# Slot weights of a fused attention and two-MoE kernel: ten parts loaded early, a ring in the order of use, filler products on TensorE

## The reference

```python
x = attention(q, k, v)          # 4 x 8 heads x 576 positions x 64, window of 128 keys, ALiBi bias
x = x.reshape(2304, 512)
# first MoE: 32 slots, 4 per expert ("slot" weights moe_w1, moe_w2)
logits = x @ phi                                  # 2304 x 32
d = softmax over tokens(logits);  slot_input = d.T @ x          # 32 x 512
for e in range(8):                                # 4 slots each
    slot_out[e] = relu(slot_input[e] @ w1[e]) @ w2[e]           # 512 x 1024, 1024 x 512
y = softmax over slots(logits) @ slot_out         # 2304 x 512
# second MoE: all tokens through all 8 experts ("big" weights moe2_w1, moe2_w2)
P = 8 Sinkhorn rounds of exp(y @ w_gate)
out = sum over e of P[:, e] * (relu(y @ w1[e]) @ w2[e])
```

## Time and profile before

| what | value |
|---|---|
| median of 3 runs | 1057.57 us (1056.58 to 1058.82) |
| the profiled execution: its time | 1057.44 us |
| its span, first to last instruction | 1055.5 us |
| outside the span | 1.94 us |
| mean granted TensorE clock | 0.969 |
| PE busy | 1005.1 us, 95% of the span |
| DMA, mean | 83 GB/s |

### The profile page before, as it was taken

One profiled execution on the slowest core, in us unless ns is written; L12 is line 12 of the kernel. 1 busy time (PEld: TensorE's weight loads), 2 busy tenths in 40 slices (PEclk: granted clock), 3 DMA queues, 4 the chain that ended last, 5 costly groups with the idle time before them and its releaser, 6 DMA issues.

```text
span 1055.5 us, 25401 instructions
## 1 busy us (share of the span) xinstructions
PE 1005.1 (95%) x8599; PEld 924.3 (88%) x8599; DVE 748.2 (71%) x1994; ACT 583.7 (55%) x1368; POOL 615.1 (58%) x522
## 2 busy tenths in 40 slices
PE   7999979579999999999999999999999999999998
PEld 5888843029999999999999999999999999999998
DVE  7767741426898867876867778778768777877675
ACT  6777710224466746555655566466546564656552
POOL 6445410004487648684966596568747873877443
PEclk9999988658999999999999999999999999999999
DMA  5773267950200220022002200210040012000111
GB/s 184 262 277 112 71 273 265 408 209 2 81 1 2 81 81 2 2 82 81 2 3 83 81 2 2 99 63 1 14 148 5 2 72 91 2 2 20 61 41 61
DMA packets 36904, 87.81 MB, mean 83 GB/s; under 512 B 2976, under 2 KB 2976, under 8 KB 36768
## 3 DMA queue, kind: packets, MB, share of 16 engines
q1 hardware_dynamic: 36768, 86.07, 22.4%
HBM read 81.35 MB, written 4.72 MB: 82 GB/s over the span
## 4 chain that ended last, share of the span: by engine, by line
PE 41%; POOL 27%; issue 22%; DMA 4%; DVE 4%; ACT 1%; POOLq 1%; ACTq 0%; DVEq 0%
POOL s_split L499 19%; PE bank L775 8%; PE bank L777 7%; PE bank L779 7%; POOL t_split L504 4%; PE bank L568 3%; PE bank L578 3%; PE bank L597 3%; DMA late_raw<-slot_w_in 3%; PE bank L725 2%; PE bank L678 2%; PE bank L615 1%; POOL raw L533 1%; POOL raw L535 1%; POOL raw L537 1%
## 5 line engine op out<-in xcount | busy, mean ns | idle before, releaser
L499 POOL TENSOR_TENSOR s_split<-s_sum,s_split 128x512 fp32r<-128x512 f32 x288 | 372.5, 1309 | 342.2 <-ACT s_split L887 337.0
L1241 DVE SCALAR_TENSOR_TENSOR acc<-bank,gate_now,acc 128x256 f32<-128x256 f32 x441 | 228.6, 519 | 146.8 <-PE bank L779 145.8
L887 ACT ACTIVATE s_split<-s_sum 128x512 fp32r<-128x512 f32 x288 | 181.8, 632 | 247.6 <-PE bank L779 137.8
L775 PE MATMUL bank<-t_split,s_split 128*128 128x256 f32 x1008 | 284.2, 282 | 1.3 <-DVE acc L1235 1.1
L777 PE MATMUL bank<-t_split,s_split 128*128 128x256 f32 x1008 | 282.6, 280 | 0.0
L779 PE MATMUL bank<-t_split,s_split 128*128 128x256 f32 x1008 | 282.6, 280 | 0.0
L775 PEld LDWEIGHTS bank<-t_split,s_split 128*128 128x128 f32 x1008 | 189.4, 188 | 5.1 <-issue 3.4
L779 PEld LDWEIGHTS bank<-t_split,s_split 128*128 128x128 f32 x1008 | 192.6, 191 | 0.0
L777 PEld LDWEIGHTS bank<-t_split,s_split 128*128 128x128 f32 x1008 | 189.4, 188 | 0.0
L775 PE MATMUL bank<-t_split,a 128*128 128x256 f32 x576 | 164.1, 285 | 5.8 <-DVE acc L1235 2.5
L777 PE MATMUL bank<-t_split,a 128*128 128x256 f32 x576 | 162.6, 282 | 0.0
(11 more groups left out here) (167 smaller groups left out, 1952.5 us busy)
## 6 DMA issues: line engine op xcount, KB each, us to landing
raw<-big_w_in SPq DMA_DIRECT2D x15, 2048.0 KB, 8.6
early_raw<-slot_w_in SPq DMA_DIRECT2D x12, 1024.0 KB, 10.5
late_raw<-slot_w_in SPq DMA_DIRECT2D x10, 1024.0 KB, 13.5
slot_raw<-slot_w_in SPq DMA_DIRECT2D x7, 1024.0 KB, 5.2
q_ring<-q_tiles SPq DMA_DIRECT2D x18, 256.0 KB, 4.6
k_ring<-k_tiles SPq DMA_DIRECT2D x18, 256.0 KB, 4.9
v_ring<-v_rows SPq DMA_DIRECT2D x18, 256.0 KB, 2.7
out_rows<-acc SPq DMA_DIRECT2D x18, 256.0 KB, 2.0
```

What stands on the lines that cost most here:

```text
L499: pool.tensor_tensor(s_split[:, i, 1, :, :], s_sum[:, i, :, :], s_split[:, i, 0, :, :].bitcast(F32), ALU.subtract)\
L775: pe.matmul(to, left[:, 0, f, :], t_place(parity, k, 0)[:, f, :], start=(f == 0 and k in FRESH), stop=False, skip_group_check=k not in FRESH)
L887: act.activation(s_split[:, i, 0, :, :], s_sum[:, i, :, :], ACT.Copy).then_inc(s_hi_ready, 1)
L1241: done = dve.scalar_tensor_tensor(out=to, in0=got, scalar=gate, in1=to, op0=ALU.mult, op1=ALU.add)
```

## The change

The masked bias copy is gone: for the two mixed tiles DVE sets the masked quarter of each score tile and reads the plain bias in two pieces. Its room and some more takes three buffers `mid_raw`, so that ten parts are loaded during attention. Three parts (`early_raw`) follow at the end of attention and four (`late_raw`) behind `x_used`: 17 buffers. From part 17 on the buffers are used again in the order in which PE frees them, from part 0's on, without those of parts 13 and 14, which hold `w2_first`, now issued behind part 23. ACT's first weight split waits until 24 parts are used. PE makes six filler products (128 columns of weights, 512 moving columns, result never read) before each of the last eight parts, four after the last part, four before it waits for the slot outputs and twelve after the first hidden blocks. On DVE the remainders of the first pair of tiles come ahead of its sums.

```diff
     RAW_RING = 7
-    EARLY_RAW = 4
-    EXTRA_RAW = 1
+    MID_RAW = 3
+    EARLY_RAW = 3
     LATE_RAW = 4
+    PREFETCHED = RAW_RING + MID_RAW
...
-        return n if n < BUFFERS else RAW_RING + (n - BUFFERS) % AGAIN
+        return n if n < BUFFERS else n - BUFFERS if n - BUFFERS < FIRST_LATE else n - BUFFERS + SKIPPED
...
-    W2_FIRST_AFTER = BUFFERS + 2
+    W2_FIRST_AFTER = BUFFERS + RAW_RING - 1
+    FILL_FROM = BUFFERS + RAW_RING
+    SKIPPED = 2
...
                 if n >= BUFFERS:
-                    sp.wait_ge(part_used, n - AGAIN + 1)
+                    sp.wait_ge(part_used, buffer_of(n) + 1)
...
                 if n == W2_FIRST_AFTER:
-                    sp.wait_ge(comb_t_ready, (TILES + 3) // 4)
+                    sp.wait_ge(part_used, FIRST_LATE + SKIPPED)
                     sp.dma_start(w2_first[:, :, :], rows_first(moe_w2[0])).then_inc(w2_loaded, 16)
...
-            pool.wait_ge(bias_ready, HEADS)
-            pool.tensor_copy(bias_mixed[:, :, :], bias[:, :, :]).then_inc(mixed_ready, 1)
-            pool.wait_ge(mixed_ready, 1)
-            pool.memset(bias_mixed[P // 2:P, :, 0:P + P // 2], MASKED / SCALE).then_inc(mixed_ready, 1)
...
+            def fill(count):
+
+                for _ in range(count):
+                    pe.matmul(bank[7][:, :], c_stack[:, 0:P], c_stack[:, 0:512], start=True, stop=True)
...
             for n in range(PARTS // 2, PARTS):
+                if n == FILL_FROM:
+                    pe.wait_ge(comb_lo_ready, (TILES + 3) // 4)
+                if n >= FILL_FROM:
+                    fill(6)
                 part_products(bank[5], hid_wide, lambda g: n % 2 * (FT // 2) + g, n, n == PARTS // 2, n == PARTS - 1)
+            fill(4)
             pe.wait_ge(rows_copied, 2)
...
+            fill(4)
             pe.wait_ge(so_split, 1)
...
             for s in range(2):
                 hidden(0, 0, 0, s, 0, 0)
+            fill_late(12)
...
             act.wait_ge(w2_loaded, 16)
+            act.wait_ge(part_used, BUFFERS + RAW_RING)
...
+                    if t % PERIOD == MIXED:
+
+                        dve.memset(scores[P // 2:P, r, n, 0:P + P // 2], -MASKED)
+                        parts = [(slice(0, P // 2), cols), (slice(P // 2, P), slice(P + P // 2, 2 * P))]
...
             for s in range(2):
+                a11_low(0, s)
+            for s in range(2):
+                a2_low(0, 0, s)
+            for s in range(2):
                 sums_first(0, 0, s, 0)
                 sums_second(0, 0, s, 0)
```

More of the change, by code:

```diff
@@ L710, in g_products, with fill_late @@
                 last.then_inc(g_ready, 1)
+            def fill_late(count):
+                for _ in range(count):
+                    pe.matmul(bank[0][:, :], c_stack[:, 0:P], c_stack[:, 0:512], start=True, stop=True)
             def hidden(e, p, parity, s, n, before):
@@ L983, in bias_pair @@
                     dve.wait_ge(probs_t_ready, GROUP_PAIRS * (g - SCORE_RING + 1))
-                biases = bias_mixed if t % PERIOD == MIXED else bias
-                if g == 2 * MIXED and p == 0:
-                    dve.wait_ge(mixed_ready, 2)
                 for n in range(2 * p, 2 * p + 2):
@@ L991, in bias_pair @@
                         dve.memset(scores[:, r, n, 0:P // 2], -MASKED)
-                    dve.tensor_tensor_reduce(
-                        out=scores[:, r, n, cols], in0=bank[n][:, cols], in1=biases[:, GROUP_HEADS * (g % 2) + n, cols],
-                        scale=-SCALE, scalar=3e38, op0=ALU.add, op1=ALU.min, accum_out=neg_max[:, r, n:n + 1]).then_inc(scores_read, 1)
+                    parts = [(slice(0, P), cols)]
+                    if t % PERIOD == MIXED:
+                        dve.memset(scores[P // 2:P, r, n, 0:P + P // 2], -MASKED)
+                        parts = [(slice(0, P // 2), cols), (slice(P // 2, P), slice(P + P // 2, 2 * P))]
+                    for rows, cs in parts:
+                        done = dve.tensor_tensor_reduce(
+                            out=scores[rows, r, n, cs], in0=bank[n][rows, cs], in1=bias[rows, GROUP_HEADS * (g % 2) + n, cs],
+                            scale=-SCALE, scalar=3e38, op0=ALU.add, op1=ALU.min, accum_out=neg_max[rows, r, n:n + 1])
+                    done.then_inc(scores_read, 1)
             def invert_sums(g):
@@ L1151, in sums_first @@
                                          op0=ALU.max, op1=ALU.add).then_inc(s_sum_ready, 1)
-                rounded, rest = [a2[:, slot, lo, blocks_f, :, :].rearrange("p f t c -> p (f t c)") for lo in range(2)]
-                dve.scalar_tensor_tensor(out=rest, in0=bank[4 + 2 * s][:, :], scalar=0.0, in1=rounded.bitcast(F32),
-                                         op0=ALU.max, op1=ALU.subtract)\
-                   .then_inc(a2_lo_ready, 1)
+                if before:
+                    a2_low(n, slot, s)
                 dve.wait_ge(s_sum_ready, 8 * n + 4 * s + 1)
@@ L1170, in sums_second @@
                                          op0=ALU.max, op1=ALU.add).then_inc(s_sum_ready, 1)
-                dve.scalar_tensor_tensor(out=a11[:, 1, blocks_f, :], in0=first_half(s)[:, :, 0, :], scalar=0.0,
-                                         in1=a11[:, 0, blocks_f, :].bitcast(F32), op0=ALU.max, op1=ALU.subtract)\
-                   .then_inc(a11_lo_ready, 1)
+                if before:
+                    a11_low(n, s)
             kept = gates[:, 0:TILES, 0:GATES]
```

73 lines of the change are left out of this document (40 added, 33 removed).

## The result

The changed kernel takes 1047.0 us (median of 4, 1046.21 to 1048.19), the kernel before 1058.11 us beside it (median of 4, 1056.58 to 1058.82). The ratio is 0.990, its 95% interval 0.9886 to 0.9915: faster by some 11 us. The forecast was -17.2 us; 1047.0 is the upper end of the range. The profiled execution took 1046.21 us, with a span of 1044.2 (before 1055.5) and a mean clock of 0.989 (before 0.969).

A forecast was written before the change was run, and what follows sets the result against it. PE, busy 95% of the span, bounds the kernel, and the load stream bounds W2. -12.5 - 2.45 - 1.45 - 0.8 = -17.2 us on 1057.44 gives 1040.3 us; 8 in 10 range 1036.5 to 1047.0.

The forecast's parts named there:

- The ring and the stream: W2's loads: first reload 9.0 us sooner and 17 units instead of 18, last part at full clock, -12.5 us.
- a step above 2.56: Sign of being wrong, last eight parts of W2: a step of fillers and part longer than the DMA's 2.56 us.
- The split of w2_first: ACT and DVE during W2: split ends at 204 us, 6 us ahead of the last part, costing nothing.
- From the last part to g: Fillers, fold and g after W2 run at full clock, 4.6 us instead of 7.05: -2.45 us.
- From g to A12: From G, the end of g, to A12's end: late fillers raise the clock, -1.45 us; new order brings nothing.
- The rival of a cold tail: After W2: stream gains as forecast, but the tail stays at low clock and fillers there cost 3.9 us: 1048, 14%.
- The start: Start of attention: without POOL's memset of the masked copy, DVE's first step is shorter, -0.8 us.
- Mixed tiles: Attention's mixed tiles: DVE's additional 0.3 us a score, 1.2 a quad, stays below its 1.46 us wait, costing nothing.
- The rival named this mechanism: Attention's mixed tiles cost: DVE loses 3 to 5 us over four quads, total 1043 to 1045, 10%.
- if PE pauses in the mixed tiles: Sign of being wrong in attention, where mixed tiles were claimed to cost nothing.
- The second MoE can't be changed: Nearly all of the span, PE busy 95%: the edits can't change it, so no gain or loss there.

The follow-up runs named there:

- experiment 4: The changed kernel with each reload of the ring waiting for seven parts more than it needs: 1057.93 us, ratio 0.9999 to the kernel before.
- experiment 5: The changed kernel with seven parts loaded in attention instead of ten, still 17 buffers: 1052.25 us, ratio 0.9948 to the kernel before.
- experiment 6: The changed kernel without any filler product, between the parts, in the tail or ahead of A11: 1051.0 us, ratio 0.9938 to the kernel before.
- experiment 3: The changed kernel with DVE's order of the first pair's remainders, and its code in the expert loop, put back as before: 1047.54 us.
- experiment 11: The changed kernel with the masked bias copy kept, nine parts loaded in attention, and POOL writing the masked quarter first: 1042.41 us.
- experiments 1 and 2: First: changed kernel with masked copy kept, nine parts loaded in attention, 1042.21 us. Second: kernel before with two-piece mixed tiles, no copy, 1062.13 us.
- Experiments 8 to 10: In order: changed kernel without twelve late fillers, 1056.42 us; with them cut to 8 columns, 1050.7; with copy kept plus 48 DVE memsets, 1044.35.

## Why the prediction was right and where it failed

The direction was right, and so was the largest mechanism. By its own steps:

**The ring and the stream: right.** -12.5 us forecast, -11.9 measured from the start of the slot parts. The late reload, put back by itself, costs 10.3 us (experiment 4), and taking the three parts out of attention 3.4 (experiment 5). The two come to more than 11.9, since each also brought a cold first step of fillers, 1.8 and 1.6 us. The seventeenth buffer was in both and had no run of its own. Of the 0.6 us missing, 0.4 are there before any filler counts: part 24 was forecast 32.0 us behind the slot parts (161.65 + 4.47 + 10 x 2.56 - 159.69) and starts 32.4 behind. The other 0.2 are the step of PE, 7 x 0.03. A part and its fillers take 2.59 us ((213.63 - 195.50) / 7) where 2.2 to 2.5 were given. That is just over the DMA's 2.56, so PE waits only for the first of the eight parts, and then PE bounds the rest. PE's timeline of narrower stretches shows the single fillers:

```profile
196.83 0.62 PE L678 MATMUL bank<-c_stack 128*128 128x512 f32 x2
...
197.07 0.62 PE L678 MATMUL bank<-c_stack 128*128 128x512 f32 x2
...
197.53 0.62 PE L678 MATMUL bank<-c_stack 128*128 128x512 f32 x2
```

They start 0.235 us apart at full clock ((197.53 - 196.83) / 3 = 0.233), the upper end of the estimate. But the first takes 0.33 (196.50 to 196.83), and the last some 0.31 until the part at 198.08: 1.58 for six in place of 1.41. The change between fillers and parts, twice in each step, costs 0.17 us, and no term stood for it. The prediction named a step above 2.56 as a sign of being wrong, and this one is 0.03 above. The 215.7 ns of the Trainium skill ("TensorE: Matmul & The Clock Gate", section "Wait — 56ns, not 53.3ns?") are not met at full clock; its 426.7 ns at the lower one are (the late fillers start 0.427 us apart).

**The split of w2_first: right.** It was forecast to end 44 us behind the start of the slot parts; ACT and DVE show it:

```profile
193.22 2.00 ACT L906 ACTIVATE t_split<-w_first 128x1024 fp32r<-128x1024 f32 x2 [11.44 <-PE bank L671]
...
202.80 4.63 DVE L1112 TENSOR_TENSOR t_split<-w_first,t_split 128x1024 fp32r<-128x1024 f32 x4
```

It ends at 207.43, 44.35 us behind 163.08 and 7 us ahead of the last part.

**From the last part to g: right.** -2.45 forecast, -2.18 measured; the fillers are longer than the copies they cover.

**From g to A12: right, and a little better than forecast.** -1.45 forecast, -2.04 measured. A11 starts at G + 10.6 (10.3 to 11.6 were given) behind fillers of which the first nine run at half clock (twelve take 4.61 us, 225.01 to 229.62) and then bring it back: A11 and A12 are 0.12 us apart from product to product, full clock. The rival of a cold tail did not come: all the fillers together are worth 4.0 us (experiment 6), the late ones 2.7 of it up to the end of A12. That the order of the remainders brings nothing was right (experiment 3).

**The start: right in direction, its size not settled.** -0.8 forecast, -0.36 in this pair of traces at v's fifth load. DVE's step that had taken 1.24 us in the earlier trace rows is short:

```profile
7.89 0.17 DVE L1017 TENSOR_SCALAR inv_sum<-row_sum 128x4 f32<-128x4 f32 x1 [0.53 <-ACT scores L826]
```

Over all traces v's fifth load comes at 24.6 us on average in the nine kernels without the copy, at 25.9 in the three that make it as before, and at 24.3 and 25.1 in the two that write the masked quarter first. That speaks for the mechanism, and for more than 0.36, but the times of single kernels overlap, and the medians of experiment 11 could not tell. The -0.48 between the twelfth and the thirteenth v load is something else, and it wasn't foreseen: that piece takes 6.2 us in every kernel with nine or ten parts loaded in attention, with or without the copy, and 6.6 to 7.1 in those with seven. Why stays open. That the two come to -0.84, near the forecast's -0.8, is luck.

**Mixed tiles: this step failed.** They were priced at nothing and cost 4.3 us, as experiments 1 and 2 show from both sides. The text took 0.3 us a score. It was 0.54, the upper bound that it gave, since the memset was reckoned as overlapped, as in the earlier trace rows, and the two passes over half the partitions as hardly longer than one. And it held the cost of each quad against the 1.46 us of the earlier trace rows, which is the wait of the tile's second quad alone. By the waits that a tile can give, 1.46 + 0.62 = 2.1 us, the upper bound of 0.55 a score would have given 2 x (8 x 0.55 - 2.1) = 4.6 us. The rival named this mechanism, with 3 to 5 us and 10%. The prediction's own sign of being wrong, "if PE pauses in the mixed tiles", came true.

**"The second MoE can't be changed": this step failed too.** PE was busy 95% of the span, but the loop's jumps back are pauses in it. DVE's pause grew by 2.3 us at each of two jumps, and g to g by some 1 us; less small gains elsewhere that makes +1.4 us net. Experiments 8 to 10 show the cause as far as it goes: how many instructions stand in an engine's list ahead of the loop decides, whatever they do. With 48 more on DVE, DVE pauses 4.5 to 4.8 us and not 2.3. With twelve products less on PE, PE pauses 5.3 us and not 2, but with 6, 48 or 68 less it pauses 1.5 to 2.1: what counts isn't more or less but where the loop comes to lie. The instruction loads fit that, since each long pause holds one round of them more than the short ones. It is not shown outright: no run moved the loop's code alone without adding or taking instructions, the view doesn't say for which engine a load is, and the lengths at which it turns were not sought.

Together: 4.3 (mixed tiles) + 1.4 (jumps) + 0.6 (stream and steps) + 0.3 (to g) - 0.6 (to A12) + 0.4 (start) - 0.5 (twelfth to thirteenth load) = 5.9 us, and by the spans the forecast was off by 17.2 - 11.3 = 5.9.

## What to carry to other kernels

When an edit saves memory by giving an engine more and smaller instructions, count each at the full duration of the nearest row, as if nothing overlapped and as if fewer partitions were no cheaper, and set the total against the sum of that engine's waits in the whole stretch, not against its longest wait. Reuse buffers in the order in which they come free: with a stream of loads as the bound, the first reload's time is the end's time, and that alone was worth 8.5 to 10 us here. And after any edit ahead of a loop, read the pause at the loop's jump back on every engine: it can cost several us for reasons that the diff doesn't show, and a few instructions more or less can take it away again. A filler that is only just shorter than the pause it fills leaves no room to win back a cold step.

## What the runs showed of the hardware that was not expected

- A loop's jump back cost PE 1.5 to 2.1 or 5.3 us and DVE 2.3 to 2.65 or 4.5 to 5.1 us, by the number of instructions ahead of the loop; on PE this went up and down again (56 fillers ahead of the loop: 5.3; with 0, 20, 62 or 68: 1.5 to 2.1). The longer pause on PE cost 3.7 to 4.5 us of the kernel's time at each jump, that on DVE about 1.
- The long pauses are the ones in which a further instruction load starts: one of q8 in PE's, four of q14 and not two or three in DVE's.
- Products of 512 columns started 0.235 us apart at a granted clock of 1.00 and 0.427 us apart at 0.50: 1.8 times as long, not twice. A change between the fillers' shape and the parts' cost some 0.1 us each way.
- A DVE pass over 64 partitions took 0.42 us, the same as over 128.
- Where the first part and its six fillers ran at a granted clock of 0.55 to 0.59 (experiments 4 and 5), they took 4.2 to 4.4 us in place of 2.6, and that loss stayed to the last part: later steps took 2.59 us and the loads came every 2.56.
